# A fused mixing layer and two feed-forward layers: the prologue's first group, the weight remainders and the first x window are made differently

## The reference, cut to what matters

```python
# x: (2, 4096, 192); weight_gen: (2, 4096, 8 heads, 7 taps)
w = softmax(weight_gen, axis=-1)
out = einsum('bshk,bskhg->bshg', w, windows_of_7(x))      # x padded with 6 zero rows ahead of each batch
# first layer, d_ff = 1536
rms = sqrt(mean(x * x, axis=-1) + 1e-6); xn = x / rms * rms_g
x = (silu(xn @ w_gate) * (xn @ w_val)) @ w_out
# second layer, d_ff = 2048
h = x @ w_in
return (h * sigmoid(1.702 * h)) @ w_out2
```

## Time and profile before

| what | us |
|---|---|
| median of 3 runs (1239.91 to 1240.71) | 1239.94 |
| the profiled execution, its own time | 1238.86 |
| its span, first to last instruction | 1237.1 |
| PE busy in the span | 1225.7 (99%) |
| DVE, ACT, POOL busy in the span | 771.5 (62%), 685.3 (55%), 65.3 (5%) |

### The profile page before, as it was taken

How to read it: one execution, slowest core, us unless ns; L and a number is a source line. 1 busy time by engine, 2 the same in 40 slices (tenths; PEclk the granted TensorE clock), 3 DMA queues, 4 the chain that set the end, 5 groups by cost and what they waited for, 6 DMA issues and landing times.

```text
span 1237.1 us, 28976 instructions
## 1 busy us (share of the span) xinstructions
PE 1225.7 (99%) x12030; PEld 1079.9 (87%) x12030; DVE 771.5 (62%) x1197; ACT 685.3 (55%) x1230; POOL 65.3 (5%) x78
## 2 busy tenths in 40 slices
PE   8999999999999999999999999999999999999998
PEld 5888889888898888989998898888999889888898
DVE  7877484865748567494764848657485674944533
ACT  6656545565554555646555455555545556464554
POOL 4524000000000000000000000000000000000000
PEclk9999999999999999999999999999999999999999
DMA  7310000000001001010010100001010010000000
GB/s 208 109 55 33 18 33 2 21 29 18 33 2 49 2 18 33 6 46 1 18 33 19 33 2 20 31 18 34 1 50 1 18 33 2 14 2 14 2 14 14
DMA packets 14769, 33.70 MB, mean 27 GB/s; under 512 B 1846, under 2 KB 7860, under 8 KB 14640
## 3 DMA queue, kind: packets, MB, share of 16 engines
q1 hardware_dynamic: 14640, 31.85, 8.1%
HBM read 25.55 MB, written 6.29 MB: 26 GB/s over the span
## 4 chain that ended last, share of the span: by engine, by line
PE 93%; ACT 2%; DVE 2%; issue 1%; DMA 1%; SPq 0%; DVEq 0%; ACTq 0%
PE up_ps L925 45%; PE acc L925 34%; PE up_ps L929 7%; PE acc L929 6%; DVE hidden L875 1%; DMA x_win<-in_x_dram 0%; DMA stage<-in_moe_w_val_dram 0%; DVE h_lo L884 0%; ACT silu L601 0%; ACT h_hi L620 0%; ACT up_w L502 0%; ACT out_w L502 0%; PE acc L1203 0%; ACT normed_all L526 0%; DVE normed_all L712 0%
## 5 line engine op out<-in xcount | busy, mean ns | idle before, releaser
L884 DVE TENSOR_TENSOR h_lo<-hidden,h_hi 128x512 fp32r<-128x512 f32 x448 | 312.8, 698 | 358.6 <-ACT h_hi L620 357.0
L620 ACT CAST h_hi<-hidden 128x512 fp32r<-128x512 f32 x448 | 278.0, 621 | 242.3 <-DVE hidden L875 231.5
L925 PE MATMUL acc<-out_w,h_hi 64*128 64x384 f32 x1024 | 302.5, 355 | 0.3 <-DVE y_f L822 0.3
L929 PE MATMUL acc<-out_w,h_hi 64*128 64x384 f32 x1024 | 302.3, 355 | 0.0
L613 ACT ACTIVATE hidden<-up_ps 128x512 f32<-128x512 f32 x256 | 152.7, 596 | 191.3 <-PE up_ps L929 191.1
L925 PE MATMUL acc<-out_w,h_lo 64*128 64x192 f32 x1024 | 255.0, 249 | 0.0
L929 PE MATMUL acc<-out_w,h_lo 64*128 64x192 f32 x1024 | 254.7, 249 | 0.0
L929 PE MATMUL up_ps<-x_hi,up_w 64*128 64x512 f32 x752 | 236.8, 394 | 0.0
L925 PE MATMUL up_ps<-x_hi,up_w 64*128 64x512 f32 x752 | 236.3, 393 | 0.0
L925 PE MATMUL acc<-h_hi,out_w 64*128 64x512 f32 x576 | 195.8, 393 | 2.3 <-issue 2.0
L929 PE MATMUL acc<-h_hi,out_w 64*128 64x512 f32 x576 | 195.8, 393 | 0.0
(11 more groups left out here) (149 smaller groups left out, 3224.5 us busy)
## 6 DMA issues: line engine op xcount, KB each, us to landing
x_win<-in_x_dram SPq DMA_DIRECT2D x14, 960.0 KB
out_dram<-out_sb SPq DMA_DIRECT2D x15, 384.0 KB, 2.3
stage<-in_moe_w_out_dram SPq DMA_DIRECT2D x13, 192.0 KB, 3.5
logits<-in_weight_gen_dram SPq DMA_DIRECT2D x16, 112.0 KB, 2.0
stage<-in_moe_w_in_dram SPq DMA_DIRECT2D x4, 256.0 KB, 3.2
stage<-in_moe_w_in_dram SPq DMA_DIRECT2D x8, 128.0 KB, 2.9
stage<-in_moe_w_gate_dram SPq DMA_DIRECT2D x3, 256.0 KB, 5.1
stage<-in_moe_w_gate_dram SPq DMA_DIRECT2D x6, 128.0 KB, 4.7
```

What stands on the lines that cost most here:

```text
L620: nc.scalar.copy(h_hi[:, u % 4, :], hidden[:, u % 2, :]).then_inc(hi_ready, 1)
L884: nc.vector.tensor_tensor(h_lo[:, u % 4, :], hidden[:, u % 2, :], h_hi[:, u % 4, :].bitcast(F32), ALU.subtract).then_inc(lo_ready, 1)
L925: return nc.tensor.matmul(ps, w[TOP], data[TOP], start=start, stop=stop)
L929: return nc.tensor.matmul(ps, w[LOW], data[LOW], start=start, stop=stop)
```

## The change

- **x(0).** The last sum of the mixing is made in two halves; ACT squares three of the four token rows, the first two of them after the first half, DVE the fourth. The epsilon is a 193rd element of each row of `mixed` (now a view with rows of 193 words, `mixed_eps`), set once by GpSimd, so that GpSimd's addition goes. ACT makes `y_hi` from PSUM in one instruction (`round_main`, scale and rounding); DVE makes the remainder of the main part from PSUM in two instructions that multiply and subtract. x(1) is made in the same way.
- **Pairs.** A "rest" chunk of gate or val holds the gate's rows on one half of the partitions and the value's on the other. The remainder of a val chunk is then both remainders, and a gate chunk has none. A rest chunk of `w_in` takes three DMAs instead of two.
- **Remainders.** TensorE makes those of chunks 0, 2 and 3 alone, ahead of `turn_x(0)`. GpSimd makes all others, from chunk 4 on, and begins when DVE has scaled group 0. It rounds chunk 5 itself. ACT rounds the others in a new order (`HI_BEHIND`), one of each unit's while it waits for DVE's product.
- **Group 1.** Its four new rows of x are loaded to `out_sb`, after chunk 8; the halo is read where group 0 left it. Taps 3 to 5 are then two multiplications each. Two of its multiplications stand ahead of block 0 (`AHEAD`), where one did.
- **SiLU's table** is loaded at the end of ACT's prologue, by an activation of one column.

```diff
-        return 32 if g == 0 else g * 16 + 64
+        return g * 16 + 32
...
-    AHEAD = ["mul0"]
-    MIX_SLOT_0 = {0: ["mul1", "mul2"], 1: ["add1", "mul3"], 2: ["add2"], 3: ["mul4"], 4: ["add3", "mul5"],
+    AHEAD = ["mul0", "mul1"]
+    MIX_SLOT_0 = {0: ["mul2"], 1: ["add1"], 2: ["mul3", "add2"], 3: ["mul4"], 4: ["add3", "mul5"],
...
-    BY_PE, FIRST_LEFT = 8, 6
-    FIRST_HI = SLOTS + LENT + 1
+    LEFT, HI_POOL = (0, 2, 3), 5
+    X_BEHIND = 9
+    HI_FIRST = 7
+    HI_BEHIND = (9, 11, 13, 15, 17, 19, 21, 21, 22, 23, 24, 26)
...
-        mixed = sb("mixed", [P, STEP, D])
+        mixed_eps = sb("mixed_eps", [P, STEP, D + 1])
+        mixed = mixed_eps[:, :, 0:D]
...
-                sp.wait_ge(tapped, TAPS)
-                sp.dma_start(x_win[:, own:, :], x_v[:, 0:HALO + STEP - own, :]).then_inc(x_in, 16)
+                sp.wait_ge(taps_summed, 1)
+                sp.dma_start(second_x, x_v[:, STEP:2 * STEP, :]).then_inc(x_in, 16)
...
+                if n == HI_POOL:
+                    pool.wait_ge(staged[place_of(n)], staged_count(n))
+                    for hi, f, _, _, _ in parts:
+                        last = nc.gpsimd.tensor_copy(hi, f)
+                    last.then_inc(own_hi, 1)
+                    pool.wait_ge(own_hi, 1)
...
-                nc.gpsimd.tensor_scalar_add(rms_stat[:, 1, :], rms_stat[:, 0, :], D * 1e-6).then_inc(summed, 1)
-                pool.wait_ge(summed, g + 1)
-                nc.gpsimd.tensor_tensor(rms_stat[:, 2, :], rms_stat[:, 1, :], neg_half[:, :],
+                nc.gpsimd.tensor_tensor(rms_stat[:, 1, :], rms_stat[:, 0, :], neg_half[:, :],
...
             rms(0)
-            pool.wait_ge(x_ready, 2)
-            for n in range(BY_PE, CHUNKS1):
-                split_chunk(n)
+            pool.wait_ge(mix, mix_count(0, "scale"))
+            for n in range(LEFT[-1] + 1, CHUNKS1):
+                if has_lo(n):
+                    split_chunk(n)
...
+                nc.scalar.activation(hi[:, :].rearrange("p (j h c) -> p j h c", j=STEP, h=2),
+                                     turned[:, :, 0:2 * P].rearrange("p h (j c) -> p j h c", j=STEP),
+                                     ACT.Copy, scale=g_main[:, :]).then_inc(x_hi_ready, 1)
...
             mix_exp(0)
-            chunk_hi_half(0)
-            for n in range(1, 4):
+            for n in range(3):
                 chunk_hi_half(n)
             copy_left(0)
             mix_square(0)
+            chunk_hi_half(3)
             copy_left(1)
+            chunk_hi_half(4)
+            act.wait_ge(g_ready, 2)
+            round_main(0)
             copy_left(2)
+            copy_twin(0)
             mix_exp(1)
...
+            nc.scalar.activation(warm[:, :], g_main[:, :], ACT.Silu)
+            chunk_hi_half(HI_POOL + 1)
             all_blocks(run)
...
+                    for h in range(2):
+                        part = lambda data: data.rearrange("p (j h c) -> p h j c", j=STEP, h=2)[:, h]
+                        ins = nc.vector.scalar_tensor_tensor(
+                            part(lo[:, :]), turned[:, h, 0:2 * P].rearrange("p (j c) -> p j c", j=STEP),
+                            g_main[:, :], part(hi[:, :].bitcast(F32)), ALU.mult, ALU.subtract)
+                    ins.then_inc(x_ready, 1)
...
-                    if i == 0 and u == 1:
-                        for n in range(FIRST_LEFT, BY_PE):
-                            leave(n)
```

More of the change, by code:

```diff
@@ L154, in staged_count, with dmas_of, has_lo, hi_count @@
     def staged_count(c):
-        return sum(32 if chunks[q][1] == "rest" else 16 for q in range(c + 1) if place_of(q) == place_of(c))
-    def even_splits(n):
-        return sum(chunks[q][0] is w_in and chunks[q][1] == "rest" for q in range(n + 1))
+        return 16 * sum(dmas_of(q) for q in range(c + 1) if place_of(q) == place_of(c))
+    def dmas_of(c):
+        w, kind, _, _ = chunks[c]
+        if kind != "rest":
+            return 1
+        return 3 if w is w_in else 2
+    def has_lo(n):
+        return chunks[n][1] != "rest" or chunks[n][2] >= U1
+    def hi_count(n):
+        return n + 1 if n < HI_POOL else n
+    def split_count(n):
+        return sum(has_lo(q) and q not in LEFT for q in range(n + 1))
     def hi_before(u):
-        if u < 0:
-            return FIRST_HI
-        return min(FIRST_HI + 2 * u + 2, CHUNKS1 + max(u - 2, 0), HELD)
+        return HI_BEHIND[u] if u >= 0 else HI_FIRST
     def chunks_for_up(m, gated):
@@ L404, in _ @@
             sp.wait_ge(x_in, x_count(0))
-            for n in range(FIRST_HI):
+            for n in range(X_BEHIND):
                 load_chunk(n)
@@ L408, in _ @@
             load_logits(2)
-            for n in range(FIRST_HI, HELD):
+            for n in range(X_BEHIND, HELD):
                 load_chunk(n)
@@ L605, in run @@
                         if i == 0 and u == TURN_1:
-                            scale_main(1)
+                            round_main(1)
+                        his = range(hi_before(u - 1), hi_before(u)) if i == 0 else ()
+                        ahead = u not in (SQUARE_0, TURN_1)
+                        for n in his[:1] if ahead else ():
+                            chunk_hi_half(n)
                     else:
@@ L621, in run @@
                     if i == 0:
-                        for n in range(hi_before(u - 1), hi_before(u)):
+                        for n in his[1:] if ahead else his:
                             chunk_hi_half(n)
@@ L710, in mix_step @@
                         dve.wait_ge(mix, mix_count(g, f"add{k - 3}"))
-                    to = mixed[:, :, :] if k == 0 else tap_at(k)
-                    ins = nc.vector.tensor_tensor(*tap_product(to, k, 0, STEP), ALU.mult)
+                    to = mixed if k == 0 else tap_at(k)
+                    for rows, first, end in tap_rows(g, k):
+                        ins = nc.vector.tensor_tensor(*tap_product(to, k, rows, first, end), ALU.mult)
                 elif step[:3] == "add":
@@ L1027, in low_pair @@
                 elif k == 3:
-                    low(a[:, :], wa[:, 2, :], rest)
+                    if i == 0 and p == 0:
+                        pe.wait_ge(x_ready, 2)
+                    low(a[:, :], wb[:, 2, :], rest)
                 elif k == 4:
@@ L1228, in _ @@
             ins.then_inc(taps_summed, 1)
-            for n in range(4):
-                leave(n)
+            for a in range(len(LEFT)):
+                leave(a)
             turn_x(0)
-            for n in range(4, FIRST_LEFT):
-                leave(n)
             before = None
```

221 lines of the change are left out of this document (111 added, 110 removed).

## The result

The changed kernel takes **1231.50 us** (median of 6 runs, 1231.38 to 1232.61) where the kernel before, run beside it, takes 1239.93 (6 runs). The profiled execution took 1231.47 us, with a span of 1229.5.

A forecast was written before the change was run, and what follows sets the result against it. TensorE was taken as the bound from 120 us on, with DVE letting it go in block 0. The transposition 3.35 us earlier gave 1238.86 - 3.4 = 1235.5, median 1236.5 us with 1.08 added; range 1235.0 to 1239.0.

The forecast's parts named there:

- equal distances from there on: After group 1's transposition at 54.6, later blocks were to take as long as before.
- The path to x(0): Prologue up to TensorE's first matmul: forecast at 19.2 instead of 21.50, 2.3 us earlier.
- the cover of 0.2: Prologue: chunk 3's `leave` was to end at 17.5, hidden because the main part is scaled at 17.7.
- DVE's lead: DVE's gain over the kernel before: 2 us at the first product (25.7), 1.7 at add6's end (50.3).
- Chunk 5's roundings: GpSimd's roundings before block 0, without a profile row: taken as 1.6 us, bounds 0.6 and 1.7.
- The hold by chunk 6: GpSimd's remainder of chunk 6, 1.30 us from 22.7, was to hold DVE's mul0 until 24.0.
- The wait ahead of step 2's fifth slot: Block 0: TensorE was to wait there over 1 us, for DVE's first product at 25.7.
- The time of the two `leave`: TensorE's 2.39 us for two `leave` in block 0 were to turn into waits for DVE, not be won.
- Lead lost: Rival: chunk 5's rounding beyond 1.6 us delays DVE; gain 2.5 to 0.1, about 1238.5 us; chance 0.21.
- GpSimd pauses at its first cast: Rival: GpSimd's first operation of a new kind begins late, delaying later remainders; 1238.0 us at 1.9 gain; chance 0.06.
- slower: Rival: DVE pays for `mixed` rows 193 words apart in every group; 1266 us at half again; chance 0.03.
- More: Rival: GpSimd seldom meets DVE, so half of 5.5 us of collisions goes; gain 5.5, 1234.4 us; chance 0.13.

The follow-up runs named there:

- `b_h_moved`: The kernel before, with 64 unused bytes a partition ahead of `h_hi`, so only `h_hi`, `h_lo` and the buffers behind them move; 1236.30 us.
- `a_rehearsed`: The changed kernel, with one more pair of matmuls on `ident` ahead of the transposition of x(0) and four behind it; 1231.46 us.
- `a_late_pool`: The changed kernel, with GpSimd starting on the weights only when DVE has made both remainders of x(0); 1232.14 us, ratio 0.9942.
- `a_moved_back`: The changed kernel, with `rms_stat` and `warm` allocated last, so buffers from `neg_half` on stand where they stood before; 1236.08 us, ratio 0.9973.
- `a_all_on`: The changed kernel, with 128 unused bytes ahead of `up_w` and 32 ahead of `neg_half`, moving weights and data; 1210.99 us, ratio 0.9767.

## Why the prediction was wrong

**The step that failed** is the first one: "from 120 us on TensorE is busy for 1113.5 of 1117 us at a granted clock of 1.00, and no edit takes a matmul out of that stretch [...] So the change acts on the prologue and block 0", and with it "equal distances from there on". The matmuls are the same, but each takes a little less time, because the new sizes of small buffers move x, y and h by 64 bytes. The whole diff holds `mixed_eps`, `normed_sq`, `rms_stat` and `warm`; I priced the rows of 193 words for DVE (the rival with 1266 us, which did not come) and not what lies behind them. With the buffers moved back the profiled time is 1235.87, against 1235.5 forecast.

**The second part of the miss** is the step from the profiled execution to the median: I added the 1.08 us by which the one of before lay under its median. That of the changed kernel lies 0.03 under its own. So of the 5.0 us missed, 4.0 are the profiled execution's (4.4 of blocks, less the 0.4 above the forecast with the buffers moved back) and 1.0 is this. A likely reason, though not shown for runs without a trace: the profiled execution of before had no fall of the clock, a fall cost that kernel 0.7 to 1.1 us at the transposition of group 1, and the changed one, in its profiled execution, nothing. The mean clocks fit: of the 19 runs of the kernel before beside `b_h_moved`, the seven at 1.000 took 1238.65 to 1239.66 us and the six at 0.998 and less 1239.44 to 1240.91.

**The path to x(0) was right:** 13.83 for the halves, 16.93 for the scaling, 19.02 for `y_hi`, 19.16 for the first matmul. Chunk 3's `leave` ended at 17.55 and stayed hidden by 0.07 us, since the main part was scaled at 17.62; the cover of 0.2 was really that thin (in `a_rehearsed`, at the lower clock, it ended at 18.55, an added pair of matmuls followed, and x(0) was transposed at 18.91).

**DVE's lead was right in sum by luck,** since two errors cancel. Chunk 5's roundings took 0.64 us and not 1.6: the lower bound was the nearer one. So GpSimd's next instruction (19.97 to 21.29) met DVE's rounding of the rest and the subtraction behind it, which the sum let run almost freely: 0.77 us for the 0.41 of `a_late_pool`, and 0.83 for 0.69. The hold by chunk 6 that the sum put on mul0 fell on `norm` of group 1 (1.35, and 0.39 in `a_late_pool`), and mul0 started at 24.34 instead of 24.0. The Trainium skill ("SBUF — State Buffer", "Who interferes with whom") has casts among the DVE instructions that can contend with GpSimd, which the prediction left as an aside. The trace agrees: the rounding is a cast, and these are its 0.77 and 0.41. The first product came 0.5 us later than forecast. The stretch from it to add6's end took 24.1 us instead of 24.6: a ninth chunk of GpSimd beside it cost some 0.2 and not 0.7.

**The wait ahead of step 2's fifth slot** was to be over 1 us and was 0.25, since TensorE itself was late: its slots between 21.6 and 24.6 took 0.42 us each at the lower clock. In `a_moved_back`, at the full clock, it is the 1.33 us shown above, as forecast. The time of the two `leave` was, as forecast, not won as such: TensorE waits ahead of 39.98 (1.44 us from start to start, for a slot of 0.23) and 0.2 us at the transposition.

**The rivals.** *Lead lost*, *GpSimd pauses at its first cast* (0.07 us lie between it and the instruction before) and *slower* did not come. *More* gave a time nearer to the result, for another reason: GpSimd meets DVE as much as before (the 24.1 us were 24.34). Its gain of 5.5 is not what its own terms give, either: 3.4 and half of 5.5 make 6.1.

## What to carry to other kernels

A change of any buffer's size moves all buffers allocated behind it, and on an engine that is busy for 99% of the time a nanosecond for each instruction decides more than a wait in the prologue. So compare the SBUF addresses of TensorE's operands of both kernels before pricing the edits, and after a run compare the distance between like marks in the steady part first. When two versions are compared for an edit, put the data at the same distance from the weights in both.

## What was not expected of the hardware

TensorE's pairs of half-height matmuls depend on where data and weights lie in SBUF relative to each other. At a distance that is a multiple of 256 bytes a block takes 73.57 us, at the others tried 74.78 to 75.17: up to 1.6 us or 2.1%. 96 unused bytes bring the kernel before from 1238.93 to 1214.30 us, more than the whole change; with the change and 160 unused bytes (`a_all_on`) it is 1210.99, faster than the kernel before by 2.3% and than the changed one by 1.7%. It was measured for fp32r, 64 rows and two streams. Which of the reads collide (a matmul's with its own weights, with the next ones or with the other stream's) was not tried; distances of 64 and 96 bytes for all operands at once neither.

The granted clock went to its 1.2 GHz level (0.50) for some 3 us (for 6 in `a_all_on`) in the first 28 us of some executions, and not in others. In the changed kernel TensorE had stood four times for 0.2 to 1.4 us between 14.76 and 21.12 before it fell; in `a_moved_back` it had stood five times for 0.2 to 0.9 us between 13.10 and 21.04, and the clock stayed at 1.00. What sets it off stays open. What it costs goes by its place: 0.7 to 1.1 us at the transposition of group 1 where it lay ahead of the first matmul of the kernel before, nothing where it lay ahead of a wait for DVE.
